# GpSimd's low parts handed to VectorE, marks shared, tiles turned behind outputs, ranks one block later

## The reference

```python
# attention: B, H, S, D = 4, 8, 576, 64
scores = causal(q @ k.T / sqrt(D)); a = softmax(scores)
out = g * (phi(q) @ M_prev) / (phi(q) @ z_prev) + (1 - g) * (a @ v)      # phi(x) = elu(x) + 1, g = sigmoid(beta)
# first mixture: N, D, E, F = 2304, 512, 8, 1024
logits = x @ w_gate + modality_bias[modality_id]
e = argmax(logits); y = softmax(logits)[e] * (relu(x @ w1[e]) @ w2[e])    # each row by its one expert
# second mixture: every row by every expert
P = exp(logits2); 8 times: rows, then columns of P divided by their sums
out = sum over e of P[:, e] * (relu(y @ w1b[e]) @ w2b[e])
```

## Time and profile before

| | |
|---|---|
| median of 3 runs | 2128.59 us (2128.15 to 2131.53) |
| profiled execution | 2126.91 us, its span 2125.3 us |
| mean granted TensorE clock | 0.997 of full speed |
| attention | 0 to about 331 us |
| first mixture | about 331 to 664 us |
| second mixture | from there to the end |
| TensorE, VectorE, ScalarE, GpSimd busy | 98%, 69%, 42%, 35% of the span |

### The profile page before, as it was taken

The page is one execution under the profiler, slowest core; times in us unless marked ns, Lnnn a source line. Parts: engine busy times, 40 slices in busy tenths (PEclk is TensorE's granted clock), DMA queues, the critical chain, the costliest instruction groups (busy, mean ns, idle before and its releaser), DMA issues.

```text
span 2125.3 us, 35431 instructions
## 1 busy us (share of the span) xinstructions
PE 2091.4 (98%) x12108; PEld 1912.4 (90%) x12108; DVE 1475.9 (69%) x2964; ACT 902.9 (42%) x2052; POOL 747.2 (35%) x651
## 2 busy tenths in 40 slices
PE   8999998999999999999999999999999999999997
PEld 7999988999998998899899889989988998998896
DVE  7877778866786866666686566666667666665663
ACT  6766755554543333343343334333334433333341
POOL 4444443111322342343245234324424432442342
PEclk9999999999999999999999999999999999999999
DMA  5522225776632222122123212211222221222120
GB/s 120 153 53 65 70 73 175 247 223 222 213 105 74 71 80 66 57 77 80 60 65 104 66 57 78 80 60 60 80 67 85 78 80 60 60 80 68 57 75 30
DMA packets 159123, 195.17 MB, mean 92 GB/s; under 512 B 77041, under 2 KB 77041, under 8 KB 158961
## 3 DMA queue, kind: packets, MB, share of 16 engines
q1 hardware_dynamic: 151360, 171.79, 27.1%
q0 software_dynamic: 6400, 20.98, 2.8%
q10 hardware_dynamic: 1200, 0.30, 0.1%
HBM read 172.04 MB, written 20.97 MB: 91 GB/s over the span
## 4 chain that ended last, share of the span: by engine, by line
PE 95%; DVE 2%; issue 1%; POOL 0%; ACT 0%; DMA 0%; SPq 0%; ACTq 0%; DVEq 0%; POOLq 0%
PE b_pso L1873 12%; PE b_pso L1874 12%; PE b_pso L1875 12%; PE b_psp L1822 11%; PE b_psp L1819 11%; PE b_psp L1821 11%; PE a_pso L649 5%; PE a_pst L636 2%; PE b_pso L1218 2%; PE b_pso L1220 2%; PE b_pso L1219 2%; PE b_psp L1218 2%; PE b_psp L1220 2%; PE b_psp L1219 2%; PE a_psp L591 2%; PE a_pss L623 1%
## 5 line engine op out<-in xcount | busy, mean ns | idle before, releaser
L1639 POOL TENSOR_TENSOR b_w2l<-b_w2r,b_w2h 128x512 fp32r<-128x512 f32 x184 | 232.0, 1293 | 881.1 <-ACT b_w2h L2058 880.8
L1873 PE MATMUL b_pso<-b_w2h,b_hh 128*128 128x512 f32 x1152 | 450.0, 391 | 1.6 <-DVE b_hl L2425 1.2
L1819 PE MATMUL b_psp<-b_x,b_ah 128*128 128x384 f32 x1344 | 450.6, 335 | 0.0
L1822 PE MATMUL b_psp<-b_x,b_al 128*128 128x384 f32 x1344 | 450.3, 335 | 0.0
L1821 PE MATMUL b_psp<-b_x,b_ah 128*128 128x384 f32 x1344 | 449.9, 335 | 0.0
L1875 PE MATMUL b_pso<-b_w2h,b_hl 128*128 128x512 f32 x1152 | 449.7, 390 | 0.0
L1874 PE MATMUL b_pso<-b_w2l,b_hh 128*128 128x512 f32 x1152 | 449.4, 390 | 0.0
L2499 DVE SCALAR_TENSOR_TENSOR b_acc<-b_pso,b_prob,b_acc 128x512 f32<-128x512 f32 x252 | 188.9, 750 | 262.6 <-PE b_pso L1875 255.3
L2094 ACT ACTIVATE b_p1u<-b_psp 128x384 f32<-128x384 f32 x96 | 46.4, 483 | 577.3 <-PE b_psp L1822 577.3
L1873 PEld LDWEIGHTS b_pso<-b_w2h,b_hh 128*128 128x128 f32 x1152 | 216.4, 188 | 46.2 <-issue 1.6
L1875 PEld LDWEIGHTS b_pso<-b_w2h,b_hl 128*128 128x128 f32 x1152 | 216.3, 188 | 45.3
(11 more groups left out here) (381 smaller groups left out, 3855.9 us busy)
## 6 DMA issues: line engine op xcount, KB each, us to landing
dense_raw<-in_moe_w SPq DMA_DIRECT2D x192, 256.0 KB, 3.8
b_w2r<-in_moe_w SPq DMA_DIRECT2D x192, 256.0 KB, 2.8
weights_raw<-in_moe_w SPq DMA_DIRECT2D x176, 256.0 KB, 4.1
y_sorted<-dense_raw SPq DMA_DIRECT2D x11, 512.0 KB, 4.1
y_sorted<-r_y POOLq DMA_DIRECT2D x22, 256.0 KB
weights_raw<-in_q SPq DMA_DIRECT2D x32, 128.0 KB, 2.5
weights_raw<-in_v SPq DMA_DIRECT2D x32, 128.0 KB, 2.6
x_tokens<-a_xs SPq DMA_DIRECT2D x4, 1024.0 KB, 4.6
```

The lines of the kernel that those rows point to most:

```text
L1639: g_.tensor_tensor(w2l[:, j, :], w2r[:, j, :], w2h[:, j, :].bitcast(F32), ALU.subtract).then_inc(s_wl, 1)
L1819: t_.matmul(bank, ah[:, i, d, col], bh[i][:, d, :], start=(first and d == 0), stop=False, skip_group_check=True)
L1822: m = t_.matmul(bank, al[:, i, d, col], bh[i][:, d, :], start=False, stop=(d == CH - 1), skip_group_check=True)
L1873: t_.matmul(o, hh[:, f, tok], w2h[:, f, :], start=(q == 0), stop=False)
```

## The change

Six parts. (1) `first_marks` on GpSimd makes ten tiles; VectorE makes the last five in one instruction, at step 28. (2) GpSimd's low parts of chunks 0 to 3 go to VectorE: at steps 38, 39 and twice behind the loop. (3) VectorE's three marks for group 1 come together behind the last head's weights, ahead of chunks 6 and 7. (4) `last_turn` stands behind a step's outputs. (5) `last_ranks` comes at f = 6, and on VectorE the last experts come ahead of the low parts of chunks 14 and 15. (6) `sources` comes behind the low parts of group 1's chunks 4 to 7, and in steps 0 and 1 of the second mixture the fourth w2 low part comes ahead of a sum.

```diff
@@ GpSimd, attention
-                for t in range(TA):
+                for t in range(2 * NI):
                     g.tensor_scalar(hotp[:, t, :], iota_p[:], posp[:, t:t + 1], None, ALU.is_equal).then_inc(s_m0, 1)
...
-            for ch in range(4):
-                c["later"]["first_weights_lo_pool"](pool, ch)
             combine(NH - 2, B - 1, H - 2)
@@ TensorE, first_sources, body and what follows it
                     if t % NI == 0:
-                        pe.wait_ge(s_m0, t + NI)
+                        if t < 2 * NI:
+                            pe.wait_ge(s_m0, t + NI)
+                        else:
+                            pe.wait_ge(s_ca, 22)
...
-                    if last and s >= 37:
-                        last_turn(s - 37)
...
                             output(b * T + s - back_by, ...)
+                    if last and s >= 37:
+                        last_turn(s - 37)
...
             turn(NH * NI - 2, *steps[-2])
+            output(NH * NI - 3, *steps[-3], NH - 1)
             last_turn(3)
-            output(NH * NI - 3, *steps[-3], NH - 1)
             turn(NH * NI - 1, *steps[-1])
@@ VectorE, first_group, body and what follows it
                 elif s == 28:
+                    t = slice(2 * NI, TA)
+                    v_.tensor_tensor(hotp[:, t, :], iota_p[:].unsqueeze(1).to_broadcast([P, NI, P]),
+                                     posp[:, t].unsqueeze(2).to_broadcast([P, NI, P]), ALU.is_equal)
...
                         first_group(b, s)
+                        if s in (38, 39):
+                            c["later"]["first_weights_lo"](dve, s - 38)
...
             turned(NH * NI - 2, *steps[-2])
-            second_marks(0)
+            c["later"]["first_weights_lo"](dve, 2)
             turned(NH * NI - 1, *steps[-1])
             weights(NH - 2, NH // 2 - 1, H - 2)
+            c["later"]["first_weights_lo"](dve, 3)
             for m in range(GT):
                 c["later"]["first_x_lo"](dve, m)
                 c["later"]["first_weights_lo"](dve, 4 + m)
             weights(NH - 1, NH // 2 - 1, H - 1)
+            for j in range(B - 1):
+                second_marks(j)
             c["later"]["first_weights_lo"](dve, 6)
             c["later"]["first_weights_lo"](dve, 7)
-            for j in range(1, B - 1):
-                second_marks(j)
             front_sums()
@@ first mixture: one semaphore for all eight w1 low parts, and the orders
-            pool.wait_ge(s_rwl0, DC)
-            pool.wait_ge(s_rwl1, DC)
+            pool.wait_ge(s_rwl0, 2 * DC)
...
-                            pe.wait_ge(s_rwl1 if f else s_rwl0, DC)
+                            pe.wait_ge(s_rwl0, DC * (f // FC + 1))
...
-                        pe.wait_ge(r["s_m0"], TA + t // NI + 1)
+                        pe.wait_ge(r["s_m0"], 2 * NI + t // NI + 1)
...
-                elif f == 5:
+                elif f == 6:
                     last_ranks()
...
             hidden_first(2)
+            hidden_first(3)
+            last_experts()
             w2_first(6)
             w2_first(7)
-            hidden_first(3)
-            last_experts()
...
-            sources()
             for ch in range(DC, 2 * FC):
                 r_weights(1, ch)
+            sources()
@@ VectorE, second mixture, hidden(k, j)
                     w2_lo(k, 2 * j)
+                    if j:
+                        w2_lo(k, 3)
...
-                if k < 2:
-                    w2_lo(k, 2 * j + 1)
+                if k < 2 and j == 0:
+                    w2_lo(k, 1)
```

More of the change, by code:

```diff
@@ L1380, in mixtures @@
         s_rwl0 = sem("first_w1_lo")
-        s_rwl1 = sem("first_w1_lo_back")
         s_rwl2 = sem("first_w2_lo")
@@ L1511, in first_weights_hi @@
             nc.scalar.activation(hi_of(ch), raw[:, ch, :], ACT.Copy).then_inc(s_rwh, 1)
[L1513 to L1516, removed]
         def first_weights_lo(dve, ch):
@@ L1522, in first_weights_lo @@
             dve.wait_ge(s_rwh, ch + 1)
-            nc.vector.tensor_tensor(lo_of(ch), raw[:, ch, :], hi_of(ch).bitcast(F32), ALU.subtract).then_inc(s_rwl1, 1)
+            nc.vector.tensor_tensor(lo_of(ch), raw[:, ch, :], hi_of(ch).bitcast(F32), ALU.subtract).then_inc(s_rwl0, 1)
         def first_turn(pe, m):
@@ L1542, in first_x_lo @@
                                     xh[:, :, m * P:(m + 1) * P].bitcast(F32), ALU.subtract).then_inc(s_rxl, 1)
-        c["later"].update(first_weights_hi=first_weights_hi, first_weights_lo_pool=first_weights_lo_pool,
-                          first_weights_lo=first_weights_lo, first_turn=first_turn,
+        c["later"].update(first_weights_hi=first_weights_hi, first_weights_lo=first_weights_lo, first_turn=first_turn,
                           first_x_hi=first_x_hi, first_x_lo=first_x_lo)
```

## The result

The changed kernel took 2119.83 us (median of 5 runs, 2119.28 to 2121.77) against 2128.15 (5 runs, 2127.01 to 2131.53) in the same comparison: a ratio of 0.9957, 95% interval 0.9943 to 0.997, faster by 8.3 us, or 0.4%. Forecast were 2122.1 us and a gain of 6.5 us.

The account below looks back on a forecast made before the run. TensorE bound the kernel, busy for 98% of the span, with a ceiling of 10.2 us. 1.5 + 2.9 + 1.3 + 0.8 = 6.5 us off 2126.91 gave 2120.4, plus 1.7 to the median 2122.1; range 2119.3 to 2127.1.

Parts of the forecast that it names:

- Part A: Marks split at step 28: GpSimd's marks stop delaying TensorE, VectorE pays one compare; 1.5 us gained, bounds 0.5 lost to 2.9.
- Part B: Steps 37 to loop end: low parts on VectorE, tiles turned behind outputs, stall goes; 2.9 us gained, bounds 1.5 to 3.6.
- Part C: First routed matmul to second product: marks together, ranks later, expert choice earlier, shorter waits; 1.3 us gained, bounds 0 to 1.7.
- Part D: Group 1's w1 second-half low parts run ahead of the sources, in VectorE's wait; 0.8 us gained, bounds 0 to 1.6.
- the 1.7 us added at the end: Last step of the sum: median of the runs shown is 1.7 us above the profiled execution, taking 2120.4 to 2122.1.
- Rival 1: Clock stays low after first sources, or falls at another place: gain 5.0 us, 2123.6 us; chance 0.20.
- What is late next is VectorE: Behind the later ranks, VectorE's places come later; its row low parts for group 1 0.2 us late at worst.
- Rival 4: Low parts don't matter, since the tail waits for the row gather issued at 316.41: gain 2.3 us, 2126.3; chance 0.05.
- Rivals 2 and 3: 2: hand-over latency in the tail, gain 3.0 us, 2125.6, chance 0.20 (latency 0.18); 3: GpSimd runs shut VectorE out, 2130.9, 0.05.

Follow-up runs that it names:

- split alone: Kernel before with only the marks split (ten by GpSimd, five by VectorE at step 28): 2127.26 us against 2128.21 for the kernel before.
- not split: Changed kernel with all 15 marks made by GpSimd again and no compare at step 28: 2120.46 us.

## Why the forecast was right or wrong

**Direction and most of the mechanism held; that the sum came near is luck.** On the profiled pair the path gave 6.83 us where the sum said 6.5. By stretch A gave 1.52 (1.5 forecast), B 3.51 (2.9), C 1.52 (1.3) and D 2.08 (0.8), 8.63 in all, less 1.80 for a wait that the prediction had put at nothing. The time was 2.3 us under the forecast. Three steps failed: what is late behind part C, the size of part D, and the 1.7 us added at the end.

**Part A (1.5 forecast).** The wait at the sources is gone, ten marks take 6.17 us (5.8), the compare 0.94 (under 0.9 was asked). Its stretch gave 1.52 us, but only 0.56 is the split: 1.2 us of waiting went, and 0.6 came back as a wait for VectorE's copy behind the compare, so VectorE did limit, as said. The other 1.0 is the fall that didn't come, and whether the split prevents it can't be said from one execution: the fall may come or not with the same wait. In the sum the split's own worth is 0.5 to 1.0. Rival 1 named the fall, and it did turn up elsewhere, with the split alone.

**Part B (2.9).** To the first routed matmul A and B gave 5.03 against 4.4, and that matmul came at 326.26 against 326.5. The subtracts were covered as argued: the parts product 0.21, L678 0.5 us. B itself gave 3.51, near its upper bound of 3.6. Undone without the lost clock, both halves are worth 2.95 us, of which the low parts are 1.7 to 2.3 and the order of the turns 0.6 to 1.2; the rest fits the mark of 0.81 us that stood ahead of the last copy, and was not undone. The prediction's own terms give 2.8, not 2.9.

**Part C (1.3) holds the step of the mechanism that failed.** `r_hidden(0)` gave 1.52, so the term looks right. But "What is late next is VectorE", 0.2 us late at worst, was wrong: it was the gather of group 1's rows, a wait of 1.60 us and a loss of 1.80. Before, its second half was issued at 344.08 and its rows turned at 352.73 without a wait; if it took 8.1 us from issue to landing, as in the changed kernel, it had some 0.5 us to spare (an estimate). The issue moved up by 3.96 us (342.54 to 338.58), the start of `r_output(0)` by 6.22: 6.22 - 3.96 - 0.5 = 1.8, which is the measured loss. Undoing the ranks showed that with this limit they are worth 0.1 in the sum, not 0.9.

**Rival 4** had the right kind of mechanism at the wrong gather: it looked at the 316.41 issue, whose rows had 11 us, and never at the next one, which no row of the prediction shows.

**Part D (0.8).** The term most mis-sized: 2.08. I left 0.5 us for the gates work and 0.2 from part C; neither came. The two waits (1.21 + 0.38) went whole, and with them 0.5 us of slow restart behind them, so even the upper bound, 1.6, the idling in the list, was too low. Moving the gates changed nothing.

**The step that failed in the time** is the last one of the sum, "the median of the runs shown is 1.7 higher", carried over to the changed kernel. The profiled execution of before (2126.91) lies under all other executions of it that were timed (2127.01 to 2135.77), with granted clocks of 0.992 to 0.997 where they are known; those of the changed kernel have 0.997 to 0.999. The medians beside each other are 0.996 (11) and 0.998 (6). So the kernel before seems to lose more clock than its one profile shows, and the changed one less. 2126.91 - 6.83 = 2120.1 with nothing added is within 0.4 of both medians (2119.83, 2120.47); with the fall at 660 us, 1.7, it is the 2121.8 of the profiled execution. That the 1.7 us is clock is argued from these clock figures, which are rounded to 0.001 (2.1 us of the span), not shown.

**Rivals 2 and 3** fell: B, C and D gave more than forecast, not less, and the compare at step 28 took 0.94 us and those beside the combine 3.36 / 3 = 1.12 us each, not a combine's length.

## What to carry over

Before crediting a sum of removed waits, list every transfer whose rows are used in the stretch behind, with its issue, its time to landing and its slack; the smallest slack caps the gain, and here it cost 1.8 of 8.6 us. Price a wait by the spacing of the instructions around it, not by its idling in the list: 1.60 us of idling was worth 2.08. Undo each part on the changed kernel, not only apply it to the old: the same ranks edit was worth 1.9 us in its stretch and 0.1 in the sum. A clock fall seen in one profile is a chance, not a term; compare sums with the lost clock taken out. And don't add the distance between a profiled execution and a median to a forecast for another kernel without knowing what it is made of.

## What the runs showed of the hardware

- GpSimd's fp32 subtracts of two operands in a row shut out VectorE's small product until the last of them ends: 0.57 us with one, 3.50 and 4.25 with four of 1.24 each (0.21 alone). The Trainium skill (SBUF — State Buffer, Who interferes with whom) has the other engine wait for one instruction; here the wait goes through the whole run of four. GpSimd's compares with a scalar let the same product through in 0.22 us. Why the marks beside a combine are only slowed (0.81 to 1.12 us) is open.
- A fall is to 0.50 of full speed, 1.2 GHz, as in the kernel before:

```profile
307.00:308.00 1.00, 1.00 (x10) 1.00 (x8) 0.90 (x4) 0.21 (x2) 0.93 (x2) 0.77 0.85 238
308.00:309.00 1.00, 1.00 (x5) 0.90 (x5) 0.15 (x1) 0.36 (x1) 0.87 (x1) 0.50 1.00 369
```

  In the six falls between step 29 and `r_output(1)` TensorE had been idle for 1.2 to 2.8 us, and the clock fell from about 0.2 us before its matmuls came back to 1.3 us after. A fall took 1.7 us of work in the kernel before and 3.4 with the split alone. Waits of the same length were followed by a fall and by none: 1.2 us (kernel before; not split) and 2.4 us (split alone; kernel before). It isn't fixed by the program either: of two executions of the changed kernel one fell at 660 to 670 us (0.84), as two of the other kernels did (0.83), and the other did not:

```profile
660.00:670.00 10.00, 8.38 (x37) 6.37 (x36) 8.39 (x24) 5.42 (x11) 0.38 (x1) 1.00 0.00 1
```

- The gather for group 1 took 8.1 us (median of its two halves) from issue to landing, in a stretch where the DMA share was 0.99 (340 to 350 us); that for group 0, of as many rows, 3.6 us with two weight loads of 256 KB in the list beside it (310 to 335 us), where the other had 18 (330 to 350). Rows of the list of DMA issues of the changed kernel, by stretch; the last number is the median from issue to landing:

```profile
a_xs<-x_tokens,idx POOLq DMA_INDIRECT x2, 3.6
```

```profile
r_xg<-x_tokens,idx POOLq DMA_INDIRECT x2, 8.1
```

  That the weight loads stretch it fits both rows. Holding them back until the gather's issue left it at 7.8 us; a kernel that holds them back until it has landed was not tried.
